# A gap of 96 bytes in SBUF ahead of the tiles that TensorE loads as weights

## What is computed

```python
# first expert stage                      # second one
h = np.maximum(x[mask] @ w1[e], 0.0)      h = np.maximum(x[mask] @ w1[e], 0.0)
out[mask] = gate_w[mask, None]*(h@w2[e])  out[mask] += top2_w[mask, k, None]*(h@w2[e])
```

## The kernel before

| tile | byte in the partition | mod 256 | minus that of W, mod 256 |
|---|---|---|---|
| ident | 16512 | 128 | 32 |
| W | 23136 | 96 | 0 |
| x_all | 154208 | 96 | 0 |
| hrow | 206016 | 192 | 96 |
| hTh, hTl | 210112, 214208 | 192 | 96 |
| xTh, xTl | 218304, 220352 | 192 | 96 |
| xrow, yrow, acc | 222400, 224448, 226496 | 192 | 96 |

## Time and profile before

### The profile page before, as it was taken

How to read it: one execution, slowest core, us unless ns; L and a number is a source line. 1 busy time by engine, 2 the same in 40 slices (tenths; PEclk the granted TensorE clock), 3 DMA queues, 4 the chain that set the end, 5 groups by cost and what they waited for, 6 DMA issues and landing times.

```text
span 728.7 us, 13666 instructions
## 1 busy us (share of the span) xinstructions
PE 661.3 (91%) x3733; PEld 533.3 (73%) x3734; DVE 351.1 (48%) x623; ACT 295.7 (41%) x443; POOL 195.6 (27%) x291
## 2 busy tenths in 40 slices
PE   2999379999999999872899999999999999999994
PEld 1888258888888888551588888888888888888883
DVE  3887674564556556117632626235244444522211
ACT  2444634464556446062522626235234444422220
POOL 2000021222122222100322434444343534433332
PEclk9999689999999999985999999999999999999998
DMA  6976777755575561452541545516336372212110
GB/s 203 373 277 222 249 258 297 244 171 205 199 240 179 195 218 44 151 183 82 173 162 58 183 148 172 185 58 227 106 90 233 95 247 68 69 58 58 44 58 19
DMA packets 40003, 118.44 MB, mean 163 GB/s; under 512 B 9533, under 2 KB 10557, under 8 KB 38413
## 3 DMA queue, kind: packets, MB, share of 16 engines
q1 hardware_dynamic: 27222, 89.51, 36.1%
q0 software_dynamic: 10608, 28.08, 11.8%
q10 hardware_dynamic: 2154, 0.60, 0.4%
HBM read 103.40 MB, written 18.43 MB: 167 GB/s over the span
## 4 chain that ended last, share of the span: by engine, by line
PE 85%; DMA 5%; DVE 4%; issue 3%; ACT 2%; POOL 0%; SPq 0%; POOLq 0%; DVEq 0%; ACTq 0%
PE bank L750 11%; PE bank L771 11%; PE bank L752 11%; PE bank L770 11%; PE bank L751 11%; PE bank L772 11%; PE bank L759 5%; PE bank L741 3%; PE bank L644 2%; PE bank L637 2%; PE bank L624 1%; DMA xrow<-x_d,picked_ids 1%; PE bank L670 1%; DVE at_row L1017 1%; DMA x_all<-x_d 1%
## 5 line engine op out<-in xcount | busy, mean ns | idle before, releaser
L750 PE MATMUL bank<-W,xTh 128*128 (+1 forms) x360 | 150.9, 419 | 5.2 <-DVE xTl L1063 2.8
L770 PE MATMUL bank<-W,hTh 128*128 x360 | 142.8, 397 | 1.4 <-DVE yrow L1079 0.8
L771 PE MATMUL bank<-W,hTh 128*128 x360 | 143.5, 399 | 0.0
L752 PE MATMUL bank<-W,xTl 128*128 (+1 forms) x360 | 143.1, 398 | 0.0
L751 PE MATMUL bank<-W,xTh 128*128 (+1 forms) x360 | 142.4, 396 | 0.0
L772 PE MATMUL bank<-W,hTl 128*128 x360 | 142.3, 395 | 0.0
L520 ACT ACTIVATE hrow<-bank 128x512 f32<-128x512 f32 x90 | 53.6, 596 | 156.9 <-PE bank L752 156.9
L524 ACT CAST hTh<-bank 128x512 fp32r<-128x512 f32 x90 | 52.8, 587 | 152.4 <-PE bank L759 152.4
L1069 DVE TENSOR_TENSOR hTl<-bank,hTh 128x512 fp32r<-128x512 f32 x90 | 62.1, 689 | 96.8 <-ACT hTh L524 96.7
L1063 DVE TENSOR_TENSOR xTl<-bank,xTh 128x512 fp32r<-128x512 f32 x47 | 32.5, 692 | 128.0 <-ACT xTh L516 128.0
L770 PEld LDWEIGHTS bank<-W,hTh 128*128 128x128 f32 x360 | 67.9, 189 | 19.0 <-issue 2.4
(11 more groups left out here) (162 smaller groups left out, 638.8 us busy)
## 6 DMA issues: line engine op xcount, KB each, us to landing
raw<-moe_w_dram SPq DMA_DIRECT2D x64, 512.0 KB, 6.1
x_all<-moe_w_dram SPq DMA_DIRECT2D x64, 512.0 KB, 6.1
qkv<-att_in_dram SPq DMA_DIRECT2D x12, 1024.0 KB, 6.8
x_d<-x_all SPq DMA_DIRECT2D x12, 256.0 KB, 7.5
out_dram<-zeros SPq DMA_DIRECT2D x1, 3072.0 KB, 13.4
x_all<-x_d SPq DMA_DIRECT2D x12, 256.0 KB, 5.9
xrow<-x_d,picked_ids POOLq DMA_INDIRECT x45, 4.1
gate_row<-gates_d,picked_gate POOLq DMA_INDIRECT x29
```

The lines of the kernel that those rows point to most:

```text
L750: pe.matmul(h_ps[half][:, :], xTh[:, k, :], hi, start=(k == 0), stop=False)
L752: last = pe.matmul(h_ps[half][:, :], xTl[:, k, :], hi, start=False, stop=(k == KD - 1))
L770: pe.matmul(y_ps[:, :], hTh[:, k, :], hi, start=(k == 0), stop=False)
L771: pe.matmul(y_ps[:, :], hTh[:, k, :], lo, start=False, stop=False)
```

## The change

```diff
         mid.close()
+        apart = (W_at + 192 - nc.sbuf_base) % 256 // 4
+        if apart:
+            sb("apart", [P, apart])
         hrow = sb("hrow", [P, 2, HF])
         hTh, hTl = sb("hTh", [P, KF, P], F32R), sb("hTl", [P, KF, P], F32R)
         xTh, xTl = sb("xTh", [P, KD, P], F32R), sb("xTl", [P, KD, P], F32R)
```

## The result

The changed kernel takes 721.64 us (median of 4 runs, 719.84 to 723.21), the kernel before on the same chip 727.46 (727.25 to 727.71): the ratio is 0.9919, interval 0.9895 to 0.9943. That is 5.8 us faster, where the prediction had 13.0 us (714.5). On another chip the same kernel had 0.9882 (0.9856 to 0.9908) of the kernel before, 8.7 us by that ratio and 9.5 by the medians. So the sign was right, and the size was too large, on the first chip by more than a factor of two.

The account below looks back on a forecast made before the run. It took TensorE's own pace in the expert loops as the bound, 2160 matmuls at 0.2343 us. With 13.0 us saved on these and all other terms at 0, 727.5 - 13.0 = 714.5 us; likeliest case's range 693 to 725.3.

Parts of the forecast that it names:

- the edit itself costs nothing: Whole kernel: no instruction, wait or DMA added, removed or moved; 96 bytes of SBUF left empty, 0 us.
- extra of 19.7 ns: Expert loops: each full-clock float32r matmul takes 0.2343 us from start to start against 0.2146, 8% more.
- the row that favoured it: Last L772 of the first expert stage, before a `keep_warm` at difference 32: 0.22 us against 0.24 at 96.
- the likeliest case: Expert loops: part of the extra goes, 1 to 16 ns a matmul; 725.3 to 693, most likely 714.5; chance 0.43.
- two reads that meet: Each of the 2160 matmuls: its stream from SBUF is held up now and then by TensorE's own weight load.
- term (a): The 2160 matmuls of the expert loops: 6 ns less for each, 13.0 us less in all.
- The upper bound: The 2160 matmuls: at best all of the 0.0197 us extra goes, 42.6 us.
- term (d): Second stage's store and fetch through `out` before VectorE's add: 0 at 13 us gain, at most 10 of 42.6.
- The row with 9.6 us of waiting for `acc`: Second stage: VectorE waits 34.2 us for `acc` in 11 cases, the longest 9.6 us.
- Nothing happens: Rival: the extra is a fixed price of float32r at full clock, addresses don't enter; 727.5 us, chance 0.25.
- It goes altogether: Rival: at 192 stream and weight load never meet; 684.9 us, or up to 695; chance 0.10.
- Slower: Rival, same weight loads: 192 may be a worse difference than 96; 740.5 us, doubled extra 770; chance 0.22.

Follow-up runs that it names:

- the sweep: Kernel before with blocks of 42 float32r matmuls appended behind the second expert stage, weights' address varied: 226.8 ns at difference 0, 234.1 at 96, 229.0 at 192.
- two kernels with the same difference: Difference 192 against the kernel before: `W` alone moved, activations at their old remainders, 724.37 us, ratio 0.9886; the changed kernel again, 724.21 us, 0.9882.

## Why the prediction was right and wrong

**What bounds the kernel, and that the edit itself costs nothing.** Right. The gain of the change is in the pace of the six lines, at the same number of instructions, in both stages; `keep_warm` kept its 0.429 us.

**That part of the extra of 19.7 ns depends on the difference.** Right, and it is a pair of addresses and not a place. But the row that favoured it, the 0.22 us of the earlier trace rows, meant nothing. The same step, the last matmul of the first expert stage before a `keep_warm`, at the same difference of 32, takes 0.23 us in the changed kernel, from here to the `keep_warm` at 299.33:

```profile
299.10 0.40 PE L775 MATMUL bank<-W,hTl 128*128 x1
```

By the starts in the eleven traces that have it at 32 it is 229 ns in two and 233 to 235 in nine. In the sweep 32 has 233.2 ns, hardly less than 96. So the likeliest case won by luck as far as this row goes; what else spoke for it was that half clock shows none of the extra. How the prediction thought of it, two reads that meet, is neither shown nor excluded.

**The size, term (a).** This is the step that failed, the 6 ns for each of 2160. In whole tiles it was 4.4 ns, 9.5 us and not 13.0, and the rest of the miss is not in the pace. In the blocks the full step from 96 to 192 is 234.1 - 229.0 = 5.1; a run of 24 matmuls between transposes does not gain it all. Averaged over all tiles from the starts in the two traces, its second to fifth distance were already short before, 231.0 ns, and are 229.9 now, and its last, to a transpose, went only from 234.1 to 233.4; the others gained the full step, 234.4 to 229.0. The upper bound, that all of the 19.7 ns was to be had, was wrong too: the best difference has 226.8, so 12 of them stayed at every difference that was tried, and only 7 to 8 depend on addresses.

**What is late next, term (d).** Put at zero for a small gain, and it was not: in the profiled pair the late steps cost 1.6 us more than before, though not in every execution. The row with 9.6 us of waiting for `acc` names the right chain, though that longest wait of all is the one at the kernel's end. The step that was missing is to take one tile with an expert's load beside it and to ask how far `yrow` is ahead of the matmul that needs its bank. Before, it was 0.42 us, with the chain already longer than the tile, and tiles that get 0.2 us shorter can use that up.

**The balance.** In the two traces: 9.5 us from the pace, 1.4 us from seven half-clock distances that the profiled execution of before had in its first tiles and the changed one had not, less 1.6 us for late steps. The remaining 0.9 us of loss up to 8.4 lies elsewhere: the first expert stage starts 1.3 us later, the stretch between the stages is 0.9 us shorter, and two steps in first tiles (at 110.29 and 350.16 us) are 0.4 us longer. Of these the 1.4 is chance and no gain: the other profiles with difference 96 have from none to 14 such distances. By the runs it is 5.8 us on this chip, and by their ratios 8.4 and 8.7 us, by two kernels with the same difference, where the kernel before takes 733 us. What parts the first chip's 0.992 from that I can't say; the intervals touch.

**The rivals.** *Nothing happens* was wrong: the pace depends on the addresses of TensorE's own two operands, 226.8 to 234.1 ns. SBUF — State Buffer of the Trainium skill, section Who interferes with whom, calls its two read ports independent, and that alone would have left 727.5; the measurement decides. The same section's word that PE never waits on anyone, taken as a word on other engines, agrees with the sweep, where TensorE alone has the paces of the full loops, 234 and 229 ns. *It goes altogether* was wrong for 192 and, as the sweep shows, for every difference: the best has 226.8. *Slower* was wrong for 192. Its worry, that 96 might be one of the good differences, was open when it was written; the sweep has 96 as the worst of all that were tried, which the argument that it already costs 8% had only guessed.

## What to carry to other kernels

Where a kernel is bound by float32r matmuls of 128 columns of weights and 512 moving columns, the addresses of weights and moving operand, mod 256, are worth a sweep: a few dozen matmuls for each difference, appended to the kernel and read by their distances, rank them all in one run, and 0 or 240 was best here. For other widths the order was another, so sweep the shape that the kernel has. Judge such an edit by the number of matmuls in a window without waits, since the gains of whole runs (5.8, 8.4 and 8.7 us for one and the same effect) scatter more than the difference between two good places. When you compare waits of two kernels in one window, see that both have the same work in it: the wait at the stage's end fell inside it for one and outside for the other here. And when a bound engine gets faster, find the serial chain that it could run into by the long waits on other engines, and read in one tile how long before the bound engine needs it the chain is done; the chain's period alone doesn't tell.

## What the runs showed of the hardware

- A float32r matmul with 128 columns of weights and 512 moving columns at full clock takes 226.8 to 234.1 ns from start to start, by the difference of the two operands' addresses mod 256; bfloat16 takes 216 at both differences that were tried.
- The dependence is fine: 0 has 226.8 ns, 4 bytes on 232.4, 8 bytes on 230.7, 240 has 227.3 and 248 has 233.4.
- With 384 moving columns it is all but gone (173.3 ns at 96, 174.0 at 0), with 256 it is 117.8 to 120.2 and 0 is the slowest of three; 11 to 14 ns over the stream's own time stay with each float32r matmul.
- Fewer columns of weights change it, but not in step with the load's length: at difference 96 it is 234.1 ns with 128 columns, 226.8 with 64 and 230.7 with 32; at 192 it is 229.0, 228.3 and 232.0.
